# Small tiles merged, weights at another distance from the x tiles, and a copy ahead of a scan

## The chip, the cores and the metric

The kernel runs on one core of one Trainium2 chip. The metric is device time in microseconds, from the start of the program to its end; lower is better.

## What is computed

A linear attention with decay over r, k, v and w, followed by two feed-forward networks on its output:

```python
# attention: 4 x 8 heads, 768 tokens, 48 channels; state is 48 x 48 for each head
cur = u * k[t] outer v[t]
y[t] = r[t] @ (state + cur)
state = w[t] * state + k[t] outer v[t]
# first network, 3072 tokens x 384, inner width 2048
h = x @ w_in
x = where(h >= 1, h, where(h <= -1, 0, (h + 1)**2 / 4)) @ w_out
# second network, inner width 1536
g = x @ w_gate
out = (silu(g) * (x @ w_val)) @ w_out2
```

## The kernel before

The 3072 tokens are cut into 8 groups of 384, each of three windows of 128. The attention of a group is done by windows with matrix products: decays come from prefix and suffix scans along the tokens on VectorE, keys and receptances are scaled with them, and TensorE forms the products within a window and the state between windows. While TensorE works through the first network of group g, the attention of group g + 1 is slipped in between its tiles, and the scans of group g + 2 run on VectorE.

Precision: each weight and each activation is split into a high and a low part (names that end in hi and lo; fp32r), and a product is the sum of three matmuls, hi x hi, hi x lo and lo x hi. A matmul has a 128 x 128 weight as its stationary operand and streams 384 columns, the tokens of a group. So a tile of the first product (tokens into 128 inner channels, L1202) is 3 x 3 matmuls, and a tile of the second product (128 inner channels into the three accumulators, L1230) is 3 x 3 as well. The second network has two first products for each tile, gate and value.

The first network has 16 tiles (J1) in each group, the second 12 (J2). The order of work on each engine is written out by hand in slots: in slot (g, j) TensorE does the first product of tile j + 2, then attention work if any is due, then the second product of tile j. ScalarE and VectorE turn the hidden tile into ghi and glo in between. ScalarE writes ghi (L806), VectorE writes glo as the residual (L1055) and updates the gate (L1062). Synchronisation is by semaphores, which only count up; engines wait for a count.

At the end of a group the three accumulators are copied into `stage`, the first three slots of the tile `ring`: accumulators 0 and 2 by ScalarE (L828), accumulator 1 by VectorE (L1067, in `copy_out`). The second product of the next group's first tile takes the accumulators in the order 0, 2, 1 and waits for these copies, for accumulator 1 on the semaphore `ed`. SP then stores `stage` to memory (L610).

On VectorE the scans (L965, a reciprocal at L968, L975) have slots of their own. In group 0 they stand in slots 11, 14 and 15 (`SCAN_SLOTS_FIRST`), in later groups in 10, 13 and 14. So in group 0 a scan and the copy share slot 15.

Tiles of SBUF are placed by hand, one behind another: `place` takes the next free byte of a partition and rounds the size up to 32 bytes. The order is x (xhi, xlo, two of each, 4,608 bytes a tile), gate, ghi, glo (two of each, 1,536 bytes a tile), ring (10,752), constants (1,024), `w_checked` (1,024), three small tiles, then the weights of the first network (each family and part 24,576 bytes) and behind them the attention's tiles. When the attention is done, the second network's weights take the place of attention tiles and of first-network weights. The three small tiles belong to a guard on the decays: `beyond` holds sums that ScalarE writes for each window, VectorE adds them into `bad` (L1001), and one matmul with `ones` (L1345) sums over partitions for a flag.

Of the kernel before, what the change touches and what calls it, by code (L numbers as in the profile page):

```python
# [24 lines left out]
F32 = mybir.dt.float32  # L25
# [15 lines left out]
PR = 64 + D  # L41
KT = DM // P
J1, J2 = FF1 // P, FF2 // P
# [30 lines left out]
OPS_CHECK = 2 * NW  # L74
# [32 lines left out]
def first(g):  # L107
    return isinstance(g, int) and g == 0
# [10 lines left out]
def fills(g):  # L119
    return FIRST_FILLS if first(g) else FILLS  # L120
# [6 lines left out]
def build_program(nc, w_d, kr_d, tok_d, u_d, cst_d, w1i_d, w1o_d, w2g_d, w2v_d,  # L127
                  w2o_d, rs_d, ks_d, vs_d, ws_d, us_d, out_d, x2_d, ys_d):
    ctx = ExitStack()
    with ctx:  # L130
        at = [nc.sbuf_base + (-nc.sbuf_base) % 32]

        def place(name, shape, dt, offset=None):

            size = 2 if dt == mybir.dt.bfloat16 else 4
            for n in shape[1:]:
                size *= n
            if offset is None:
                offset = at[0]
                at[0] += (size + 31) // 32 * 32  # L140
            assert offset + size <= nc.sbuf_usable_end, (name, offset + size)
            return nc.alloc_sbuf_tensor_at(name, shape, dt, offset=offset), offset + size


        xhi = [place(f"xhi{i}", [P, KT, T], F32R)[0] for i in range(2)]
        xlo = [place(f"xlo{i}", [P, KT, T], F32R)[0] for i in range(2)]
        gate = [place(f"gate{i}", [P, T], F32)[0] for i in range(2)]
# [2 lines left out]
        ring, _ = place("ring", [P, KT + RING2, T], F32)  # L150
        stage = ring[:, 0:KT, :]
        cst, _ = place("cst", [P, 2 * P], F32)
# [1 line left out]


        checked, _ = place("w_checked", [PR, NPAIR * WIN], mybir.dt.bfloat16)
        beyond, _ = place("w_beyond", [PR, 2, OPS_CHECK + 2], F32)
        bad, _ = place("w_bad", [PR, OPS_CHECK + 1], F32)
        ones, _ = place("ones", [PR, 9], F32)
        ones = ones[:, 0:1]  # L160


        flag_at = (nc.sbuf_usable_end - 4) // 32 * 32
        flag, _ = place("flag", [1, 1], mybir.dt.int32, flag_at)
        w1_at = at[0]
        assert w1_at % 64 == 32
        w1i = [place(f"w1i{n}", [P, J1, KT * P], F32R)[0] for n in ("hi", "lo")]
        w1o_at = at[0]
        w1o = [place(f"w1o{n}", [P, J1, DM], F32R)[0] for n in ("hi", "lo")]
# [3 lines left out]
        w_at, _ = place("w_by_channel", [PR, NW, WROW + 1], F32)  # L173
        suf, _ = place("suf", [PR, NW, WROW], F32)
        kr, _ = place("k_r_by_channel", [PR, NW, 2, NPAIR, WIN], F32)
        last, _ = place("last_of_segment", [PR, WROW], F32)
        seed, _ = place("scan_seed", [PR, WROW], F32)
        tok, _ = place("r_k_v_by_token", [P, NW, 3, DM], F32)
        uu, _ = place("u_rows", [P, DM], F32)
# [3 lines left out]
        st, _ = place("state", [PR, NPAIR, D], F32)  # L183
        xn, _ = place("x_by_token", [P, NW, DM], F32)
        ring_b, _ = place("ring_b", [P, RING - KT - RING2, T], F32)
        dg, _ = place("diag", [P, NW, H], F32)
# [24 lines left out]
        for j in range(NA, J2):  # L211
            n = 2 + 6 * (j - NA)
# [50 lines left out]
        def state_pairs(w, parity):  # L263

            return 1 if parity == 1 and w == NW - 1 else NPAIR
# [22 lines left out]
        def bank_of(g, f):  # L288

            return (attb + hid + acc)[f % 8] if isinstance(g, int) and g == 0 else attb[f % NBANK]  # L290

        def twin(g, w):

            return (g * NW + w) % 2

        def y_two_ago(g, w):

            g2, w2 = divmod(g * NW + w - 2, NW)
            return g2 * NF + fill_no(g2, "Y", w2) + 1

        def cols(w):
            return slice(w * WIN, (w + 1) * WIN)
# [653 lines left out]
        def _(e):  # L956
# [61 lines left out]
            def drain(g, f, parity):  # L1018
                kind, w, n = fills(g)[f]
                src = bank_of(g, f)  # L1020
                if kind == "AT":
                    if n == 0:
                        decay_state(g, w, parity)
                    if first(g):
                        e.wait_ge(ld["cst"], 16)
                        e.wait_ge(zero_p, 9)
                    if g * NW + w >= 2:
                        e.wait_ge(fill, y_two_ago(g, w))
                    e.wait_ge(fill, g * NF + (f + 1))
                    mask = later.bitcast(U32).rearrange("p (a t) -> p a t", a=1).to_broadcast([P, 4, WIN])  # L1030
                    e.copy_predicated(att[twin(g, w)][n][:, :, :], mask, src[:, :].rearrange("p (a t) -> p a t", a=4))\  # L1031
                        .then_inc(at_out, 1)
                elif kind == "ST":
                    if first(g) and w == 0:
                        return
                    e.wait_ge(fill, g * NF + (f + 1))
                    e.wait_ge(st_dec, OPS_DECAY * (g * NW + w + 1))
                    n_pair = state_pairs(w, parity)
                    for i in range(2):
                        r0, c0 = 64 * i, D * i  # L1040
                        rows, pairs = slice(r0, r0 + D), slice(0, n_pair)
                        ps = src[rows, 0:n_pair * D].rearrange("p (a c) -> p a c", a=n_pair)
                        e.tensor_tensor(st[rows, pairs, :], ps, sbar[twin(g, w)][rows, pairs, c0:c0 + D], ALU.add).then_inc(st_out, 1)
                elif kind == "Y":
                    e.wait_ge(fill, g * NF + (f + 1))
                    e.wait_ge(diag_v, g * NW + w + 1)
                    e.tensor_tensor(xn[:, w, :], src[:, 0:DM], tok[:, w, 0, :], ALU.add).then_inc(y_out, 1)
                elif kind == "XT":
                    e.wait_ge(xh_out, g * NW + (w + 1))
                    e.tensor_tensor(xlo[parity][:, :, cols(w)], src[:, 0:DM].rearrange("p (k t) -> p k t", k=KT),  # L1050
                                    xhi[parity][:, :, cols(w)].bitcast(F32), ALU.subtract).then_inc(xl_out, 1)
# [12 lines left out]
            def copy_out(ph, g):  # L1064
                e.wait_ge(M["out", ph], (g + 2) * J[ph])
                e.wait_ge(M["st", ph], (g + 1) * 16)
                e.tensor_copy(stage[:, 1, :], acc[1][:, 0:T]).then_inc(M["ed", ph], 1)  # L1067
# [54 lines left out]
            def nxt(g, j, J_):  # L1122
                return (g, j) if j < J_ else (g + 1, j - J_)

            def slot(g, j, parity, next_half, after_next):
                last = isinstance(g, int) and g == NG - 1
                if not (last and j + 1 >= J1):
                    lo(1, *nxt(g, j + 1, J1))
                else:
                    lo(2, 0, 0)  # L1130
                if first(g) and j == XT_FIRST:
                    for f in win_slots(g)[j]:
                        drain(g + 1, f, 1 - parity)
                if not (last and j + 2 >= J1):
                    knee(*nxt(g, j + 2, J1))
                else:
                    swiglu(0, j + 2 - J1)
                if first(g):
                    if j in SCAN_FIRST:
                        scan_window(1, SCAN_FIRST[j])  # L1140
                    if j in SCALE_FIRST:
                        scale_window(1, SCALE_FIRST[j])
                    if j in DIAG_FIRST:
                        diag_sum(1, DIAG_FIRST[j])
                    if j == 6:
                        sum_w(1)
                elif next_half:
                    if j in SCALE_SLOTS:
                        scale_window(g + 1, SCALE_SLOTS[j])
                    if j in DIAG_SLOTS:  # L1150
                        diag_sum(g + 1, DIAG_SLOTS[j])
                if next_half and not (first(g) and j == XT_FIRST):
                    for f in win_slots(g).get(j, ()):
                        drain(g + 1, f, 1 - parity)
                if after_next:
                    if j in scan_slots(g):
                        scan_window(g + 2, scan_slots(g)[j])
                if after_next and j == SUM_SLOT:
                    sum_w(g + 2)
                if j == J1 - 1:  # L1160
                    copy_out(1, g)
                if last and j == 10:
                    split_x(0, 0)
                if last and j == 2:
                    e.wait_ge(w_sum, NG + 1)
                    e.tensor_reduce(bad[:, OPS_CHECK:OPS_CHECK + 1], bad[:, 0:OPS_CHECK], AX.X, ALU.add).then_inc(w_sum, 1)
                if last and j == 5:
                    e.wait_ge(w_tot, 1)
                    e.tensor_scalar(flag[:, :], attb[2][0:1, 0:1], 0.0, None, ALU.is_gt).then_inc(w_sum, 1)
# [253 lines left out]
```

## Time and profile before

| | |
|---|---|
| median of 3 runs | 992.36 us (992.11 to 992.6) |
| the profiled execution's own time | 992.52 us |
| its span, first to last instruction | 990.6 us |
| TensorE busy | 972.9 us, 98%, 6886 matmuls |
| VectorE busy | 519.5 us, 52% |
| ScalarE busy | 402.3 us, 41% |
| GpSimd busy | 163.5 us, 17% |
| data moved | 59.52 MB, mean 60 GB/s |

Busy time counts an instruction from its start to its end, and matmuls overlap each other, so TensorE's busy share tells that it always has something in flight and not how fast it goes. The pace is read from the distance of starts, or from the chain of work that ended last, in which each piece lasts until the next begins.

### The profile page before, as it was taken

The numbers are of one execution on the slowest core, as the hardware profiler recorded it, in microseconds if no ns is written. First come the engines' busy times: TensorE is split into PE (matmuls) and PEld (weight loads), VectorE is DVE, ScalarE is ACT, GpSimd is POOL, SyncE is SP. The second block draws the span as 40 slices with busy tenths as digits, with TensorE's granted clock in tenths as the row PEclk, the third lists the DMA queues.
The fourth block names the chain that finished last, engine by engine and source line by source line (L and its number), as shares of the span: only waits on it lengthen the run. The fifth ranks groups of instructions, "written<-read, shape, count | busy, mean of one in ns | idle before, by whom it ended". The sixth has DMA issues, their size and how long they took to land.

```text
span 990.6 us, 17480 instructions
## 1 busy us (share of the span) xinstructions
PE 972.9 (98%) x6886; PEld 954.7 (96%) x6886; DVE 519.5 (52%) x906; ACT 402.3 (41%) x841; POOL 163.5 (17%) x155
## 2 busy tenths in 40 slices
PE   6999999999999999999999999999999999999998
PEld 5899999999999999999999999999999999999997
DVE  8996666657576575764444433434333343334332
ACT  5665455454554554544665322222222222222222
POOL 6992210301102112020263200000000000000000
PEclk9999999999999999999999999999999999999999
DMA  9724212121222212100332100010100001010000
GB/s 303 238 66 132 85 55 86 53 86 52 87 77 62 87 43 95 68 2 1 132 108 88 57 17 32 1 49 1 48 0 29 19 0 48 0 48 0 24 1 25
DMA packets 23492, 59.52 MB, mean 60 GB/s; under 512 B 2688, under 2 KB 12032, under 8 KB 23424
## 3 DMA queue, kind: packets, MB, share of 16 engines
q1 hardware_dynamic: 23424, 58.59, 18.2%
q8 instruction: 46, 0.75, 0.3%
q14 instruction: 22, 0.18, 0.1%
HBM read 49.14 MB, written 9.44 MB: 59 GB/s over the span
## 4 chain that ended last, share of the span: by engine, by line
PE 94%; DVE 3%; issue 1%; ACT 1%; DMA 0%; DVEq 0%
PE bank L1202 50%; PE bank L1230 35%; PE bank L1258 2%; PE bank L1280 2%; PE bank L1275 1%; PE bank L1250 1%; DVE suf L965 1%; PE bank L1286 1%; PE bank L1267 1%; DVE att L1031 0%; DVE k_r_by_channel L990 0%; DVE k_r_by_channel L987 0%; DMA w_by_channel<-in_w_channel 0%; DVE glo L1055 0%; DVE gate L1062 0%
## 5 line engine op out<-in xcount | busy, mean ns | idle before, releaser
L806 ACT ACTIVATE ghi<-gate 128x384 fp32r<-128x384 f32 x224 | 117.3, 523 | 186.7 <-DVE gate L1074 95.6
L1055 DVE TENSOR_TENSOR glo<-gate,ghi 128x384 fp32r<-128x384 f32 x224 | 133.7, 597 | 113.2 <-ACT ghi L806 111.0
L1072 DVE TENSOR_TENSOR gate<-bank,gate 128x384 f32<-128x384 f32 x96 | 53.5, 557 | 223.2 <-ACT gate L925 223.2
L1202 PE MATMUL bank<-xhi,w2gv_alo 128*128 128x384 f32 x480 | 162.6, 339 | 0.0
L1202 PE MATMUL bank<-xlo,w2gv_ahi 128*128 128x384 f32 x480 | 162.5, 339 | 0.0
L1202 PE MATMUL bank<-xhi,w2gv_ahi 128*128 128x384 f32 x480 | 162.5, 339 | 0.0
L925 ACT ACTIVATE gate<-bank 128x384 f32<-128x384 f32 x96 | 47.3, 493 | 235.8 <-PE bank L1202 235.8
L1230 PE MATMUL bank<-ghi,w1ohi 128*128 128x384 f32 x384 | 134.8, 351 | 2.0 <-DVE ring L1067 1.1
L1202 PE MATMUL bank<-xhi,w1ihi 128*128 128x384 f32 x384 | 130.3, 339 | 1.3 <-issue 0.8
L1062 DVE SCALAR_TENSOR_TENSOR gate<-bank,gate 128x384 f32<-128x384 f32 x128 | 71.1, 555 | 112.4 <-ACT gate L815 112.4
L1230 PE MATMUL bank<-glo,w1ohi 128*128 128x384 f32 x384 | 130.0, 338 | 0.0
L1202 PE MATMUL bank<-xlo,w1ihi 128*128 128x384 f32 x384 | 129.9, 338 | 0.0
L1230 PE MATMUL bank<-ghi,w1olo 128*128 128x384 f32 x384 | 129.9, 338 | 0.0
L1202 PE MATMUL bank<-xhi,w1ilo 128*128 128x384 f32 x384 | 129.8, 338 | 0.0
L813 ACT ACTIVATE gate<-bank 128x384 f32<-128x384 f32 x128 | 62.8, 491 | 98.2 <-PE bank L1202 97.4
L1230 PE MATMUL bank<-ghi,w2ohi 128*128 128x384 f32 x288 | 97.5, 339 | 0.0
L1230 PE MATMUL bank<-ghi,w2olo 128*128 128x384 f32 x288 | 97.5, 339 | 0.0
L1230 PE MATMUL bank<-glo,w2ohi 128*128 128x384 f32 x288 | 97.5, 339 | 0.0
L1202 PEld LDWEIGHTS bank<-xhi,w2gv_ahi 128*128 128x128 f32 x480 | 90.0, 188 | 0.0
L1202 PEld LDWEIGHTS bank<-xlo,w2gv_ahi 128*128 128x128 f32 x480 | 90.0, 188 | 0.0
L1202 PEld LDWEIGHTS bank<-xhi,w2gv_alo 128*128 128x128 f32 x480 | 90.0, 188 | 0.0
L707 POOL TENSOR_TENSOR r_k_v_by_token<-r_k_v_by_token,diag 128x384 f32<-128x384 f32 x24 | 26.9, 1121 | 311.8 <-DVE diag L995 311.7
(95 smaller groups left out, 1580.4 us busy)
## 6 DMA issues: line engine op xcount, KB each, us to landing
r_k_v_by_token<-in_rkv_token SPq DMA_DIRECT2D x24, 576.0 KB, 5.0
k_r_by_channel<-in_kr_channel SPq DMA_DIRECT2D x24, 448.0 KB, 4.0
w_by_channel<-in_w_channel SPq DMA_DIRECT2D x24, 226.2 KB, 2.6
x_t<-ring SPq DMA_DIRECT2D x8, 576.0 KB, 2.8
x_raw<-x_t SPq DMA_DIRECT2D x8, 576.0 KB, 4.0
ring<-in_w_out SPq DMA_DIRECT2D x22, 192.0 KB, 2.5
out_t<-ring SPq DMA_DIRECT2D x7, 576.0 KB, 3.1
ring<-in_w_gate SPq DMA_DIRECT2D x12, 192.0 KB, 2.4
```

The costliest lines, as they stand in the source:

```text
L707: e.tensor_tensor(tok[:, w, 0, :].rearrange("p (h d) -> p h d", d=D), tok[:, w, 2, :].rearrange("p (h d) -> p h d", d=D), d_b, ALU.mult).t ...
L806: e.activation(ghi[j % 2][:, :], gate[j % 2][:, :], ACT.Copy).then_inc(M["hi", ph], 1)
L813: e.activation(q, hid[j % 2][:, 0:T], ACT.Relu, bias=0.5, scale=0.5).then_inc(M["q", 1], 1)
L925: e.activation(gate[j % 2][:, :], hid[j % 2][:, 0:T], ACT.Sigmoid).then_inc(M["q", 2], 1)
L965: e.tensor_tensor_scan(suf[:, w, ::-1], w_at[:, w, :0:-1], last[:, ::-1], 0.0, ALU.mult, ALU.max).then_inc(scan, 1)
L1055: e.tensor_tensor(glo[j % 2][:, :], gate[j % 2][:, :], ghi[j % 2][:, :].bitcast(F32), ALU.subtract)\
L1062: e.scalar_tensor_tensor(q, hid[j % 2][:, 0:T], 1.0, q, ALU.max, ALU.min).then_inc(M["g", 1], 1)
L1072: e.tensor_tensor(q, hid[j % 2][:, 0:T], q, ALU.mult).then_inc(M["t", 2], 1)
L1202: m = e.matmul(out, w_of(a, k), x_of(b_, k), start=start and i == 0, stop=stop and i == total - 1)
L1230: m = e.matmul(acc[k][:, 0:T], wo[a][:, j, k * P:(k + 1) * P], gs[b_][:, :], start=(j == 0 and i == 0), stop=(j == J[ph] - 1 and i == 2))
L1258: m = e.matmul(o[:, p * WIN:(p + 1) * WIN], kr[r, w, 0, p, :], kr[r, w, 1, p, :], start=True, stop=True)
L1280: m = e.matmul(out[t, h * D:(h + 1) * D], att[twin(g, w)][h % 2][:, h // 2, t], tok[:, w, 2, h * D:(h + 1) * D], start=(row_start and h == 0),
```

## The change

The three small tiles become one, `w_sums`, of 20 numbers, and `beyond`, `bad` and `ones` are parts of it. The weights are placed 96 bytes past the first x tile, counted by 256, with filler if needed; the test of the old place by 64 goes. On VectorE, in the last slot of group 0, the copy of accumulator 1 is issued ahead of the scan; in the other groups the order stays.

```diff
--- before.py
+++ after.py
@@ -142,6 +142,7 @@
             return nc.alloc_sbuf_tensor_at(name, shape, dt, offset=offset), offset + size
 
 
+        xhi_at = at[0]
         xhi = [place(f"xhi{i}", [P, KT, T], F32R)[0] for i in range(2)]
         xlo = [place(f"xlo{i}", [P, KT, T], F32R)[0] for i in range(2)]
         gate = [place(f"gate{i}", [P, T], F32)[0] for i in range(2)]
@@ -154,16 +155,18 @@
 
 
         checked, _ = place("w_checked", [PR, NPAIR * WIN], mybir.dt.bfloat16)
-        beyond, _ = place("w_beyond", [PR, 2, OPS_CHECK + 2], F32)
-        bad, _ = place("w_bad", [PR, OPS_CHECK + 1], F32)
-        ones, _ = place("ones", [PR, 9], F32)
-        ones = ones[:, 0:1]
+        sums, _ = place("w_sums", [PR, 3 * OPS_CHECK + 2], F32)
+        beyond = sums[:, 0:2 * OPS_CHECK].rearrange("q (b n) -> q b n", b=2)
+        bad, ones = sums[:, 2 * OPS_CHECK:3 * OPS_CHECK + 1], sums[:, 3 * OPS_CHECK + 1:3 * OPS_CHECK + 2]
+
+
+        W_STEP = 256
+        at[0] += (xhi_at + 96 - at[0]) % W_STEP
 
 
         flag_at = (nc.sbuf_usable_end - 4) // 32 * 32
         flag, _ = place("flag", [1, 1], mybir.dt.int32, flag_at)
         w1_at = at[0]
-        assert w1_at % 64 == 32
         w1i = [place(f"w1i{n}", [P, J1, KT * P], F32R)[0] for n in ("hi", "lo")]
         w1o_at = at[0]
         w1o = [place(f"w1o{n}", [P, J1, DM], F32R)[0] for n in ("hi", "lo")]
@@ -1152,12 +1155,14 @@
                 if next_half and not (first(g) and j == XT_FIRST):
                     for f in win_slots(g).get(j, ()):
                         drain(g + 1, f, 1 - parity)
+                if j == J1 - 1 and first(g):
+                    copy_out(1, g)
                 if after_next:
                     if j in scan_slots(g):
                         scan_window(g + 2, scan_slots(g)[j])
                 if after_next and j == SUM_SLOT:
                     sum_w(g + 2)
-                if j == J1 - 1:
+                if j == J1 - 1 and not first(g):
                     copy_out(1, g)
                 if last and j == 10:
                     split_x(0, 0)
```

## Rows read from the trace of the kernel before

**Rows 1.** The page: busy time of the engines, and TensorE's granted clock by slices.

```profile
PE 972.9 (98%) x6886; PEld 954.7 (96%) x6886; DVE 519.5 (52%) x906; ACT 402.3 (41%) x841; POOL 163.5 (17%) x155
...
PEclk9999999999999999999999999999999999999999
```

**Rows 2.** The page: the chain that ended last, by line.

```profile
PE bank L1202 50%; PE bank L1230 35%; PE bank L1258 2%; PE bank L1280 2%; PE bank L1275 1%; PE bank L1250 1%; DVE suf L965 1%; PE bank L1286 1%; PE bank L1267 1%; DVE att L1031 0%; DVE k_r_by_channel L990 0%; DVE k_r_by_channel L987 0%; DMA w_by_channel<-in_w_channel 0%; DVE glo L1055 0%; DVE gate L1062 0%
```

**Rows 3.** The chain in order of time (start, duration, what), second network.

```profile
529.62 3.18 PE bank L1202 x18
532.80 1.59 PE bank L1230 x9
...
978.00 3.18 PE bank L1202 x18
```

**Rows 4.** Groups by line: busy us, mean ns of one; one group of each three.

```profile
L1202 PE MATMUL bank<-xhi,w2gv_ahi 128*128 128x384 f32 x480 | 162.5, 339 | 0.0
...
L1230 PE MATMUL bank<-ghi,w1ohi 128*128 128x384 f32 x384 | 134.8, 351 | 2.0 <-DVE ring L1067 1.1 <-DVE glo L1055 0.9
L1202 PE MATMUL bank<-xhi,w1ihi 128*128 128x384 f32 x384 | 130.3, 339 | 1.3 <-issue 0.8 <-DVE gate L1062 0.5
...
L1230 PE MATMUL bank<-ghi,w2ohi 128*128 128x384 f32 x288 | 97.5, 339 | 0.0
...
L1202 PE MATMUL bank<-xhi,w2gv_bhi 128*128 128x384 f32 x96 | 32.5, 339 | 0.0
```

**Rows 5.** The chain in order of time, first network, group 1.

```profile
103.22 1.59 PE bank L1202 x9
104.81 1.59 PE bank L1230 x9
```

**Rows 6.** The waits: who waited for whom, us in total, times, longest.

```profile
PEld bank L1230 <- DVE ring L1067: 1.5, 1, 1.5
...
PE bank L1230 <- DVE ring L1067: 1.1, 1, 1.1
```

**Rows 7.** Groups by line: the instructions on the small tiles.

```profile
L1001 DVE TENSOR_TENSOR w_bad<-w_bad,w_beyond 112x6 f32<-112x6 f32 x8 | 2.3, 284 | 0.0
...
L1345 PE MATMUL bank<-ones,w_bad 112*1 112x1 f32 x2 | 0.2, 164 | 0.0
```

**Rows 8.** The chain in order of time: transposes of keys and of the attention's output.

```profile
111.17 0.39 PE bank L1250 x4
...
151.76 0.33 PE bank L1286 x3
```

**Rows 9.** The timeline of VectorE, end of group 0 (start, duration, engine, line, operation).

```profile
98.68 0.55 DVE L1062 SCALAR_TENSOR_TENSOR gate<-bank,gate 128x384 f32<-128x384 f32 x1
99.15 1.22 DVE L965 TENSOR_TENSOR_SCAN suf<-w_by_channel,last_of_segment 112x516 f32<-112x516 f32 x1
...
100.69 1.23 DVE L975 TENSOR_TENSOR_SCAN w_by_channel<-w_by_channel,scan_seed 112x516 f32<-112x516 f32 x1
101.84 0.53 DVE L1067 COPY ring<-bank 128x384 f32<-128x384 f32 x1
102.28 0.55 DVE L1055 TENSOR_TENSOR glo<-gate,ghi 128x384 fp32r<-128x384 f32 x1
```

**Rows 10.** The timeline of TensorE, end of group 0 and first tile of group 1.

```profile
98.30 0.34 PE L1230 MATMUL bank<-ghi,w1olo 128*128 128x384 f32 x1
...
100.77 0.34 PE L1230 MATMUL bank<-glo,w1ohi 128*128 128x384 f32 x1
100.95 0.33 PE L1230 MATMUL bank<-ghi,w1olo 128*128 128x384 f32 x1
102.42 0.44 PE L1230 MATMUL bank<-ghi,w1ohi 128*128 128x384 f32 x1 [1.14 <-DVE ring L1067]
102.70 0.34 PE L1230 MATMUL bank<-glo,w1ohi 128*128 128x384 f32 x1
```

**Rows 11.** The timeline of SP's DMA issues, end of group 0.

```profile
102.44 0.37 SPq L610 DMA_DIRECT2D x_t<-ring  x1
104.53 3.52 SPq L555 DMA_DIRECT2D w_by_channel<-in_w_channel  x2
```

## The prediction

> **What bounds the kernel.** I read the page's first two parts first. TensorE is busy 98% of the span, and its granted clock is 0.9 or more in every one of the 40 slices, so it runs at the upper of its two levels, 2.4 GHz, from end to end [rows 1]. The reader is to see that no other engine can be the bound: VectorE has 52%, ScalarE 41%. The chain that ended last says the same by line: L1202 (the first product of a tile) and L1230 (the second) hold 85% of the span, and the other lines of TensorE hold most of the rest [rows 2].
>
> Next I read the chain in order of time. In the second network it is nothing but pieces of 18 and 9 matmuls, 3.18 and 1.59 us long. From the piece at 529.62 to that at 978.00 lie 448.38 us, which is 94 slots of 4.77 us, each with 27 matmuls: 448.38 / (94 x 27) = 176.67 ns for a matmul of 384 columns [rows 3]. At one column per cycle of 2.4 GHz these columns last 160.0 ns, so each matmul carries 16.7 ns that its columns don't explain. How many there are comes from the groups by line, of which I show one of each three: 3 x (480 + 384 + 384 + 288 + 96) = 4896 [rows 4]. So one nanosecond on such a matmul is 4.9 us of the time, and the unexplained part is 4896 x 16.7 ns = 81.6 us. The first network's pieces of nine last the same 1.59 us [rows 5].
>
> Last I read the waits. TensorE waited once for VectorE's copy at L1067, for 1.1 us by its matmul and 1.5 us by its weight load [rows 6]; no later wait of TensorE is as long.
>
> **Part 1: where the tiles lie.** The three small tiles took 64 + 32 + 64 = 160 bytes of a partition; one tile of 20 numbers, 80 bytes, is rounded up to 96. What lies between the first x tile and these tiles (x, gate, ghi, glo, ring, constants, w_checked) is 40,448 bytes, which is 158 x 256. So the weights began 160 bytes by 256 past the x tiles; they now begin 96 past, and the filler that the new line adds is 0 bytes. Every weight tile, and x, ghi and glo as well, is a whole number of 256 bytes long, so all 4896 matmuls change from one distance to the other together. Tiles behind the weights move by the same 64 bytes; among themselves their distances stay.
>
> The instructions on the small tiles stay as many and as large: 8 additions of 284 ns and the matmul of one number at L1345, 164 ns [rows 7]. Their addresses and the step from one half of the sums to the other (8 numbers, now 6) change, and I cost that at nothing: VectorE, which does the additions, is idle 48% of the span. If that cover were gone they would cost at most their 2.3 us.
>
> The price of the new distance is not in the trace, since every large matmul in it has the old one. The bounds: the 16.7 ns vanish (81.6 us less), or as much again comes on top (81.6 us more). Nothing excludes either sign. The nearest rows are the transposes of the attention: they too load a stationary tile while another operand streams, and they have two other distances. By the sizes of the tiles k_r_by_channel lies 32 bytes by 256 past the identity that streams against it, and x_by_token 96. Four transposes of 112 columns lasted 0.39 us, three of 128 columns 0.33 us, so 0.87 and 0.86 ns a column at the two distances [rows 8]. They show no effect of the distance, and I take 0 ns. They are plain float32 at half the pace in columns, though, so they don't rule an effect out.
>
> The Trainium skill has two rules that pull apart here. "TensorE: Matmul & The Clock Gate", section "Step-by-step: what each phase is for", says that weights and the streaming operand are read through independent ports, so that a load doesn't slow the matmul that runs; by it the distance is worth nothing, the sum that I take. The same page's section "Wait — 56ns, not 53.3ns?" gives a warm matmul its columns at 2.4 GHz and about 2.5 ns; for 384 columns that would be 162.5 ns, which the measured 176.67 ns contradicts by 14.2 ns. By that second rule the 14.2 ns have a cause of their own, and a change that removed them would be worth 69.4 us, an estimate from that page's figure.
>
> **Part 2: the copy ahead of the scan.** In group 0, tile 15, VectorE did its scans (99.15 to 101.84), then the copy of accumulator 1 (101.84, 0.53 us) [rows 9]. TensorE needed the copy for the first tile of group 1: its matmul before the wait starts at 100.95, the next at 102.42, the one behind it at 102.70 [rows 10]. So the stall is 1.47 - 0.18 = 1.29 us, and 0.28 - 0.18 = 0.10 us more until weights load under matmuls again: 1.39 us. The copy's own condition, the last matmul of group 0, starts at 98.30 and lasts 0.34 us, so it is met at about 98.7. VectorE is then in the update of a gate that starts at 98.68 and lets the next instruction start at 99.15. The copy will start there without a wait and end by 99.7, against 101.13 when TensorE asks for it. The whole 1.39 us goes.
>
> What is late next? The scans come 0.5 us later, and the residual behind them (L1055, 102.28) starts when it started before, since the same work stands ahead of it [rows 9]. It ends at about 102.85. The matmuls that need it began at 104.81 [rows 5]; 1.39 us sooner they begin at 103.42, still 0.6 us behind it. Nobody asks for the scans' results before the next group. The copy issues no transfer, but the store of x that it releases on SP's queue left at 102.44 and can now leave near 99.7; the next issue there stands at 104.53, so nothing is queued behind it sooner [rows 11]. After that the chain is TensorE alone, so the gain lasts to the end.
>
> **The sum.** Profiled execution 992.52 us, its span 990.6, 1.9 us around it; the median is 992.36. 0 - 1.39 us from 992.36 gives 991.0 us. This is 0.14% less, below the 0.2% (2.0 us) that a measurement of this kernel can tell from no change.
>
> **The rivals.**
> - The new distance takes a part of the 16.7 ns away, 0.5 to 6 ns. For it: the part exists, nothing else in the trace names its cause, and the transposes at other distances have 3 to 4 ns over a cycle of 1.2 GHz per column (110 against 106.7, 97.5 against 93.3). Against it: matmuls on xhi, xlo, ghi and glo against five families of weights all have the same 176.7. 2 ns give 991.0 - 9.8 = 981.2 us; the ends are 988.6 and 961.6. From 0.13 ns on it counts as faster.
> - It takes most of it away, 6 to 16.7 ns: 961.6 to 909.4 us. Only the bound speaks for so much.
> - It adds to it, the other side: at L1202 and L1230 each matmul waits longer for an operand. 2 ns give 1000.8 us, the bound 1072.6. It decides from 0.69 ns on (1.39 + 2.0 us over 4896). No row shows a streaming matmul above 176.7, while rows show less per column, so this has less chance than the gain.
> - The copy's gain doesn't appear, since something else holds TensorE at the same place (the residual behind the scans, if they take longer in their new place): 992.4 us. Against it stand the 0.6 us.
>
> **How the numbers follow.** Forecast without an effect of the distance, 0.37; a part taken away 0.31; most taken away 0.14; added 0.13; gain of the copy lost 0.05. The predicted time is that of the first, 991.0 us, its own range 990.5 to 991.6. The range over the cases runs from 962 (all of the second case) to 1005 us (2.9 ns added); it leaves out the 0.14 and about 0.04 of the slower case. Faster by over 0.2%: 0.31 + 0.14, and 0.02 of the first case if the time falls by 0.6 us more than its sum, 0.47. Slower: 0.13. Within: 0.40.
>
> **What would show it.** The copy: L1067 at about 99.2, and TensorE's wait for it gone. The distance: pieces of 18 and 9 matmuls in the second network's chain of 3.18 and 1.59 us if it is worth nothing; each 0.01 us on a piece of nine is 1.1 ns on a matmul and 5.4 us on the time. The prediction is wrong if these pieces change, or if a new wait of TensorE stands between 99 and 107 us.

## The result, and the profile after

The changed kernel takes 976.13 us (median of 4 runs, 975.88 to 976.46) against 992.24 us before (4 runs): a ratio of 0.9838, 95% interval 0.9821 to 0.9855. So 16.1 us are gone, 1.6%. The time lies inside the stated range of 962 to 1005 us, but it is not that of the likeliest case: it is the first rival's, a part of the unexplained nanoseconds taken away.

The page of the changed kernel: busy time and the granted clock, then the costliest groups of TensorE that answer to [rows 4].

```profile
PE 958.0 (98%) x6886; PEld 940.0 (96%) x6886; DVE 517.8 (53%) x906; ACT 401.5 (41%) x841; POOL 163.4 (17%) x155
...
PEclk9999999999999999999999999999999999999999
...
L1207 PE MATMUL bank<-xhi,w2gv_ahi 128*128 128x384 f32 x480 | 161.3, 336 | 0.0
...
L1235 PE MATMUL bank<-ghi,w1ohi 128*128 128x384 f32 x384 | 133.8, 349 | 0.9 <-DVE glo L1058 0.9
...
L1235 PE MATMUL bank<-ghi,w2ohi 128*128 128x384 f32 x288 | 96.8, 336 | 0.0
```

The lines have moved down by up to five (L1202 is now L1207, L1230 is L1235, the copy L1067 is L1070). Counts, clock and TensorE's 98% are as in [rows 1], so this is no change of work or of clock. A matmul lasts 336 ns instead of 339, and the copy is no longer among what the second product waited for. Since matmuls overlap, the pace has to be read from the chain. The chain of the changed kernel in order of time, second network:

```profile
521.62 3.12 PE bank L1207 x18
524.74 1.56 PE bank L1235 x9
...
961.54 3.12 PE bank L1207 x18
```

These are the pieces of [rows 3], 3.12 and 1.56 us long where they were 3.18 and 1.59. From 521.62 to 961.54 lie 439.92 us, again 94 slots of 27 matmuls: 173.33 ns a matmul, 3.33 ns less than 176.67. Both are means. By the starts of single matmuls in the trace of the second network, the changed kernel's lie 173 or 174 ns apart throughout, while before they lay 174, 180, 175 and 178 ns apart, again and again in steps of four matmuls (within 1 ns). The operands repeat in steps of three (hi x hi, hi x lo, lo x hi), so the added time does not belong to one kind of product.

The first network's part is shorter than the count suggests. Two rows of the same chain:

```profile
45.38 1.80 PE bank L1235 x9
...
102.76 1.56 PE bank L1235 x9
```

The piece at 45.38 stood at 45.49 before: up to here the chain goes mostly through VectorE and ScalarE, and faster matmuls hardly help. The piece at 102.76 stood at 104.81 [rows 5], 2.05 us later; 1.4 us of this is the copy. The timeline of VectorE at the end of group 0:

```profile
98.21 0.55 DVE L1065 SCALAR_TENSOR_TENSOR gate<-bank,gate 128x384 f32<-128x384 f32 x1
98.67 0.55 DVE L1070 COPY ring<-bank 128x384 f32<-128x384 f32 x1
99.14 1.22 DVE L968 TENSOR_TENSOR_SCAN suf<-w_by_channel,last_of_segment 112x516 f32<-112x516 f32 x1
...
101.83 0.53 DVE L1058 TENSOR_TENSOR glo<-gate,ghi 128x384 fp32r<-128x384 f32 x1
```

The copy follows the gate at once, the scan follows the copy, and the residual at 101.83 is in good time for the second product that starts at 102.76.

### The profile page after: what moved, and what is told of

The parts are those of the page before. It is cut to its first block, busy times and chain, and to the rows that moved or that the text cites. A ratio compares the mean times of both kernels' runs of the same rounds, so it can differ in the third digit from the quotient of the medians.

```text
span 974.3 us, 17480 instructions
## 1 busy us (share of the span) xinstructions
PE 958.0 (98%) x6886; PEld 940.0 (96%) x6886; DVE 517.8 (53%) x906; ACT 401.5 (41%) x841; POOL 163.4 (17%) x155
## 4 chain that ended last, share of the span: by engine, by line
PE 96%; DVE 1%; DMA 1%; issue 1%; ACT 0%; SPq 0%; DVEq 0%; ACTq 0%
PE bank L1207 50%; PE bank L1235 36%; PE bank L1263 2%; PE bank L1285 2%; PE bank L1280 2%; PE bank L1255 1%; PE bank L1291 1%; PE bank L1272 1%; DMA w_by_channel<-in_w_channel 1%; DVE suf L968 0%; PE bank L1252 0%; DVE glo L1058 0%; DVE gate L1065 0%; DVE w_by_channel L978 0%; DVE k_r_by_channel L993 0%
## 5 line engine op out<-in xcount | busy, mean ns | idle before, releaser
L1207 PE MATMUL bank<-xhi,w2gv_ahi 128*128 128x384 f32 x480 | 161.3, 336 | 0.0
L1207 PE MATMUL bank<-xlo,w2gv_ahi 128*128 128x384 f32 x480 | 161.3, 336 | 0.0
L1207 PE MATMUL bank<-xhi,w2gv_alo 128*128 128x384 f32 x480 | 161.3, 336 | 0.0
L1235 PE MATMUL bank<-ghi,w1ohi 128*128 128x384 f32 x384 | 133.8, 349 | 0.9 <-DVE glo L1058 0.9
L1207 PE MATMUL bank<-xhi,w1ihi 128*128 128x384 f32 x384 | 129.2, 336 | 1.4 <-issue 0.8
L1235 PE MATMUL bank<-glo,w1ohi 128*128 128x384 f32 x384 | 129.1, 336 | 0.0
L1207 PE MATMUL bank<-xhi,w1ilo 128*128 128x384 f32 x384 | 129.1, 336 | 0.0
L1207 PE MATMUL bank<-xlo,w1ihi 128*128 128x384 f32 x384 | 129.0, 336 | 0.0
L1235 PE MATMUL bank<-ghi,w1olo 128*128 128x384 f32 x384 | 129.0, 336 | 0.0
L1235 PE MATMUL bank<-ghi,w2ohi 128*128 128x384 f32 x288 | 96.8, 336 | 0.0
L1235 PE MATMUL bank<-ghi,w2olo 128*128 128x384 f32 x288 | 96.8, 336 | 0.0
L1235 PE MATMUL bank<-glo,w2ohi 128*128 128x384 f32 x288 | 96.8, 336 | 0.0
L1207 PEld LDWEIGHTS bank<-xhi,w2gv_ahi 128*128 128x128 f32 x480 | 90.2, 188 | 0.0
L1207 PEld LDWEIGHTS bank<-xlo,w2gv_ahi 128*128 128x128 f32 x480 | 90.2, 188 | 0.0
L1207 PEld LDWEIGHTS bank<-xhi,w2gv_alo 128*128 128x128 f32 x480 | 90.2, 188 | 0.0
```

The lines of the kernel that those rows point to most:

```text
L1207: m = e.matmul(out, w_of(a, k), x_of(b_, k), start=start and i == 0, stop=stop and i == total - 1)
L1235: m = e.matmul(acc[k][:, 0:T], wo[a][:, j, k * P:(k + 1) * P], gs[b_][:, :], start=(j == 0 and i == 0), stop=(j == J[ph] - 1 and i == 2))
```

## Experiments

The theory: the distance, by 256 bytes, between the weights and the operand that streams against them sets the pace of every large matmul, and the copy adds 1.4 us. Rivals: the merged tile did it; the weights' own address did it; 96 is good because operands that lie far apart collide less. "Second network" below is the pace of its chain, worked out as above from the start of one slot to that of a later one.

**Each part alone.** The first kernel has the weights back at 160:

```diff
-        at[0] += (xhi_at + 96 - at[0]) % W_STEP
+        at[0] += (xhi_at + 160 - at[0]) % W_STEP
```

> The changed kernel with its weights put back to 160 bytes past the x tiles (by 256); the merged small tile and the moved copy stay. Theory A (the distance between weights and the streaming operand sets the pace of every large matmul): pieces of 9 matmuls return from 1.56 to 1.59 us, and only the copy's gain is left, 992.24 - 1.4 = 990.9 us. Theory B (something else of the edit, the merged tile or the smaller step between its halves, makes the matmuls faster): pieces stay at 1.56 us and the time near 976.1 us. If the copy's gain is eaten by a later wait, 992.2 us.

It took 991.35 us (11 runs) against 992.74 us (15 runs) of the kernel before on the same chip, a ratio of 0.9987 (0.9978 to 0.9996): 1.39 us. Its chain, in order of time, has the old pieces, but no stall among them:

```profile
98.60 1.59 PE bank L1207 x9
100.19 1.59 PE bank L1235 x9
101.78 1.59 PE bank L1207 x9
103.37 1.59 PE bank L1235 x9
```

and its timeline of VectorE shows the copy at 99.11, the first scan 0.42 us later than before, and the residual where it was [rows 9]:

```profile
99.11 0.55 DVE L1070 COPY ring<-bank 128x384 f32<-128x384 f32 x1
99.57 1.22 DVE L968 TENSOR_TENSOR_SCAN suf<-w_by_channel,last_of_segment 112x516 f32<-112x516 f32 x1
...
102.27 0.53 DVE L1058 TENSOR_TENSOR glo<-gate,ghi 128x384 fp32r<-128x384 f32 x1
```

So the merged tile, which this kernel keeps, is worth nothing that can be told: the time falls by what the stall was worth, and the pieces are the old ones. The second kernel has the new distance and the old order:

```diff
-                if j == J1 - 1 and first(g):
-                    copy_out(1, g)
                 if after_next:
                     if j in scan_slots(g):
...
-                if j == J1 - 1 and not first(g):
+                if j == J1 - 1:
                     copy_out(1, g)
```

> The changed kernel with VectorE's copy put back behind the scan; the new distance stays. Theory A: the pace stays at 1.56 us for 9 matmuls, TensorE waits again for the copy in group 0, and the time is 976.1 + 1.4 = 977.5 us. If the copy is worth nothing once the matmuls are faster, 976.1 us.

It took 977.38 us (5 runs), a ratio of 0.9847 (0.9834 to 0.9861), 15.4 us less than the kernel before. Its waits show the old stall again, a little longer, since TensorE now comes sooner:

```profile
PEld bank L1233 <- DVE ring L1070: 1.6, 1, 1.6
PE bank L1233 <- DVE ring L1070: 1.3, 1, 1.3
```

Its chain in order of time, behind that stall, shows something more:

```profile
104.06 1.59 PE bank L1233 x9
105.66 1.59 PE bank L1205 x9
...
125.22 1.56 PE bank L1233 x9
126.79 1.56 PE bank L1205 x9
```

The distance is 96 from end to end, and yet TensorE runs at the old pace for about 80 large matmuls, until 118 us; from 122 us on, behind more of the attention's work, it is back at 1.56 us. So the good distance does not exclude the slow pace, and the distance alone does not set it.

15.4 us and 1.4 us make 16.8, against 16.1 measured together; the runs of one kernel spread over 0.6 to 1.4 us, so the two add up as far as can be told.

**Distance or address.** Every tile lies 64 bytes further up, x included, so that the weights are at the old address by 256 and at the new distance:

```diff
+        at[0] += 64
         xhi_at = at[0]
```

> The changed kernel with every tile, x included, 64 bytes further up; the distance stays 96. The weights are then at the same address by 256 as in the kernel before. Theory A (the distance counts): 1.56 us for 9 matmuls, about 976 us. Rival (the weights' own address by 256 counts, not the distance): 1.59 us, about 991 us.

976.73 us in a single run, with the changed kernel's pieces in the chain. At this one shift the distance counts, and the weights' address alone does not.

```profile
564.22 3.12 PE bank L1208 x18
567.34 1.56 PE bank L1236 x9
```

**Other distances.** The same line as in the first experiment, with another number. The kernels below differ in it alone, apart from the one at 112.

> Distance 224 instead of 96, else as the changed kernel. If the distance counts by 128, it acts as 96 does: 1.56 us for 9 matmuls, 976 us. If it counts by 256, another pace; the kernel before had 160, so a pace between or beyond 1.56 and 1.59 us tells that the period is longer than 128. No theory here gives its size; one cycle of 1.2 GHz on each matmul is 4.1 us.

> Distance 0 by 256. Theory A as the runs so far have it: distance 96 gives 173.3 ns a matmul (208 cycles of 1.2 GHz), 160 gives 176.7 ns (212), 224 both of them in one run. Theory A1, loads and stream collide more often the nearer they lie: more than 212 cycles, 1000 us or above. Theory A2, only the half of 64 bytes counts beside a lock of the two streams: 212 cycles, 991 us.

> Distance 32 by 256, the last one that is 32 by 64. Theory A2 (a lock into one of two patterns): 173.3 or 176.7 ns, so 976 to 991 us, with no pace outside. Theory A1 (nearness): slower than distance 160, above 991 us.

> Distance 64 by 256. A1: between 32 and 96, so below 991 us. A2: the distances 0 and 64 by 64 behave as distance 0 does.

> Distance 192 by 256. So far 0, 32 and 96 give 173.33 ns a matmul in the second network, 64 gives 174.67, 160 and 224 give 176.67. Theory of a half (distances from 0 to 127 are good, from 128 on bad, with 64 in between by a mixed pattern): 176.67 ns, 985 to 991 us. Theory that only 160 and 224 are bad, the 32 by 64 class in the upper half: 173.33 ns, 976 us.

> Distance 128 by 256, the last of the eight steps of 32. So far 0, 32, 96 and 192 give 173.33 ns in the second network, 64 gives 174.67, 160 and 224 give 176.67. If slow distances go with the lower or the upper half by 256, 192 has already spoken against it. If every distance that is a multiple of 64 avoids 176.67 ns: 173.33 or 174.67 ns, 976 to 983 us. If 128 belongs with its neighbour 160: 176.67 ns, 986 to 991 us.

`place` gives addresses in steps of 32 bytes only. For 112, x, ghi and glo became slices of one tile, 16 bytes into it:

```diff
+        SH = 16 // 4
+        moving, _ = place("moving", [P, 4 * KT * T + 4 * T + 8], F32R)
+
+        def part(n, size):
+            return moving[:, SH + n:SH + n + size]
...
-        at[0] += (xhi_at + 96 - at[0]) % W_STEP
+        at[0] += (xhi_at + 16 + 112 - at[0]) % W_STEP
```

> x, ghi and glo start 16 bytes into one common tile, so that the weights are 112 past them, a distance between the steps of 32 tried so far. If only steps of 32 bytes matter: 173.33 ns and 976 us. If 16 bytes matter, another pace; a pace below 173.33 ns would make this kernel faster than both, each cycle of 1.2 GHz by 4.1 us, down to 160.0 ns (911 us) at the most.

| distance by 256 | us | second network, ns a matmul |
|---|---|---|
| 0 | 976.33 | 173.3 |
| 32 | 977.16 | 173.3 |
| 64 | 982.26 | 174.7 |
| 96 (the changed kernel) | 976.13 | 173.3 |
| 112 | 982.50 | 174.7 |
| 128 | 986.48 | 175.6 |
| 160 (copy alone) | 991.35 | 176.7 |
| 192 | 976.04 | 173.3 |
| 224 | 986.71 | 176.7 |

Apart from 96 and 160 these are single runs, on four chips on which the kernel before took 992.45 to 992.92 us. At 0 both expected times were missed, at 192 the second theory was met (173.33 ns, 976 us), and at 128 the pace lies between the two that were named. At 112 the pace is another one, but there the streaming operands also begin 16 bytes off a multiple of 32, so this row is not the distance alone. Nearness fails as an explanation: 0 and 32 are as good as 96, 64 between them is not. So do halves of 256 (192 is good), the class by 64 bytes (32 and 96 are good, 160 and 224 are not), and a period of 128 (96 and 224 differ). And 96 is nothing special: four of the eight steps of 32 have the same best pace in the second network, and none tried is below it. What the old place had was the slowest pace of all. How a pace is read, at 128 for example: its chain has the same piece of nine at 534.27 and at 932.43, 84 slots apart, and 398.16 / (84 x 27) = 175.6 ns.

```profile
534.27 1.58 PE bank L1235 x9
...
932.43 1.58 PE bank L1235 x9
```

The kernel at 224 shows more. Its second network has the slow pace, but its total is 4.6 us better than at 160. Rows of its chain in order of time, first network, two stretches:

```profile
149.51 0.33 PE bank L1291 x3
149.84 1.56 PE bank L1235 x9
151.40 1.56 PE bank L1207 x9
...
170.12 1.56 PE bank L1207 x9
171.68 0.39 PE bank L1255 x4
...
212.12 0.33 PE bank L1291 x3
212.45 1.59 PE bank L1235 x9
214.04 1.59 PE bank L1207 x9
...
233.12 1.59 PE bank L1207 x9
234.71 0.38 PE bank L1255 x4
```

The reader is to see both paces in one kernel, on the same lines and the same weights. Each stretch starts behind three transposes of the attention and runs unbroken for 22 us until the attention breaks in again; the first keeps 1.56 us for nine all the way, the second 1.59. So at this distance there are two patterns. They change from group to group: by the starts in the trace, the long stretches that begin near 150, 275 and 401 us have the fast one, those near 212, 338 and 463 us the slow one. Three transposes of the same kind stand ahead each time, so what chooses the pattern stays open. The kernel at 64 is mixed too, with stretches at 173.3, 174.7 and 176.7 ns, while at 160 every unbroken stretch of 35 matmuls or more was slow. The whole second network is one such stretch, so for 64 and 224 the table's pace is that of the pattern which this one run happened to keep.

**Which operands.** The low parts of the gate and value weights of ten of the twelve tiles lie 64 bytes further, at 160:

```diff
-            t, o = place(f"w2gv_a{n}", [P, NA, 2, KT * P], F32R, o)
+            t, o = place(f"w2gv_a{n}", [P, NA, 2, KT * P], F32R, o + (64 if n == "lo" else 0))
```

> Distance 96 for all but the low parts of ten of twelve gate and value tiles, which lie at 160. They are 480 of the 4896 stationary operands, and each is loaded while xlo streams. If the pace is set by the pair of operands that are read at once, these 480 times cost 4 cycles more, 1.6 us: 977.7 us, and the second product (L1235) stays at 1.56 us for 9. If a lock once lost stays lost, the second network falls to 1.59 us for 9 in its streaming part and the time goes to about 984.8 us (2592 matmuls by 3.33 ns). If only the weights' own matmul counts, 977.7 us too, but the longer gap is the one from the low part to the next high part.

975.69 us, and the chain still has pieces of 3.12 and 1.56 us:

```profile
563.35 3.12 PE bank L1207 x18
566.47 1.56 PE bank L1235 x9
```

All three expectations missed: one load in three of the second network's first product at the old distance costs nothing that this single run shows; the 1.6 us that were expected would have taken it to 977.7 us. In the last kernel ghi and glo are moved behind the attention's tiles, so that the first product has distance 96 and the second 160:

```diff
-        ghi = [place(f"ghi{i}", [P, T], F32R)[0] for i in range(2)]
-        glo = [place(f"glo{i}", [P, T], F32R)[0] for i in range(2)]
...
         dg, _ = place("diag", [P, NW, H], F32)
+        at[0] += (w1_at - 160 - at[0]) % W_STEP
+        ghi = [place(f"ghi{i}", [P, T], F32R)[0] for i in range(2)]
+        glo = [place(f"glo{i}", [P, T], F32R)[0] for i in range(2)]
```

> Distance 96 between weights and x, as in the changed kernel, but ghi and glo lie so that the weights are 160 past them: the first product (L1207) has the new distance, the second (L1235) the old one. If the pace is set by the pair of operands of the matmul at hand: L1235 at 1.59 us for 9, L1207 at 1.56; 1632 second-product matmuls by 3.33 ns make 976.1 + 5.4 = 981.5 us. If a streak must be long for the slow pattern to settle, the nine of L1235 stay near 1.56 and the time near 976 us. If the slow pattern, once there, stays, all go to 1.59 us and 991 us.

982.82 us. Its chain in order of time has the old pace in the second product and nearly the new one in the first:

```profile
562.98 3.13 PE bank L1208 x18
566.10 1.59 PE bank L1236 x9
567.69 3.13 PE bank L1208 x18
570.81 1.59 PE bank L1236 x9
```

So the slow pace came back in the runs of nine that have the old distance, although weights and x lie as in the changed kernel: the pair of weights and streaming operand counts, not the weights' place against other tiles. The time is 1.3 us over the 981.5 us worked out for this case, and no run says why.

## Why the prediction was right or wrong

- What bounds the kernel: right. From group 1 on (103 us) the chain holds TensorE alone, and a nanosecond on each large matmul was worth nearly what was worked out. Of 4.9 us a nanosecond, 3.33 ns would make 16.3 us; the layout alone gave 15.4. The second network gave its full 2592 x 3.33 ns = 8.6 us, the first 6.7 of 7.7 us, since its first tiles hang on VectorE and ScalarE and some 80 matmuls behind the stall kept the slow pace.
- The copy: right in each step. 1.39 us was the sum and 1.39 us the measurement of it alone, though the interval of that measurement runs from 0.4 to 2.2 us, so that the two agree to the digit is luck; the copy starts without a wait, the scan comes 0.42 us later (0.5 was said), the residual keeps its time, and the store leaves at 99.30 in the changed kernel (near 99.7 was said).
- The merged tile at nothing: right as far as can be told, as the kernel with the copy alone shows.
- The distance at nothing: this step failed. The likeliest case priced it at 0 ns, and it was worth 3.33 ns on a matmul of the second network and 15.4 us in all; by the prediction's own sign, the changed pieces, that case was wrong. The price came from the nearest rows, the transposes at distances 32 and 96 [rows 8], and these rows can't show it. The transposes move against the identity together with the weights: in the kernel at 224, x_by_token lies 160 past the identity, the distance at which the large matmuls are slow throughout, and three transposes still last 0.33 us (149.51 above). The prediction had left this open, since they run at half the pace in columns. The one thing the rows did show, 16.7 ns that the columns don't explain, spoke for the first rival, which had been given 0.31. The argument against that rival was empty: that all pairs of operands have the same 176.7 ns says nothing on the distance, as by the prediction's own count they all have the same one. The rival's range of 0.5 to 6 ns held the 3.33 ns; its worked time of 981.2 us took 2 ns. That the measured time lies inside the stated range comes from this rival, not from the sum.
- Most of the 16.7 ns taken away: wrong. At 173.33 ns there are still 13.3 ns over 160.0, and no distance tried changed that.
- The other side, an added cost: not seen; no distance of the nine is slower than 176.7 ns in the second network, so the old place left none of them worse.
- The two rules of the Trainium skill ("TensorE: Matmul & The Clock Gate"). By the section "Step-by-step: what each phase is for", a load of weights doesn't slow the matmul that runs; with the copy's effect taken out, moving the weights against the stream changed the large matmuls by 3.33 ns in the mean, so the operands' places do count, and here the measurement decides; that the load itself is what slows the stream is not shown. The section "Wait — 56ns, not 53.3ns?" has the columns and 2.5 ns, by an estimate from that figure 162.5 ns here; the best pace of these runs is 10.8 ns above it, and no run here, each with a load for every matmul, shows what the rest is.

What stays open is the mechanism. That two reads of one part of the memory collide would fit the dependence on the distance, but no run takes the load of weights away or looks at a single read, and the order of good and bad distances (0, 32, 96, 192 good) was not derived from anything. The trace has a load of 128 x 128 weights at 188 ns, before and after alike, longer than the pace of either kernel; so the loads may hold some of the 13.3 ns that are left, which no run tests. What chooses between the patterns at one distance is open as well. A period of 256 was not tested either: the kernels compared lie within one such step.

## What to carry to other kernels

Work out what a streaming matmul's columns last at the granted clock, and set the distance of starts beside it: what is left over, times the count, is the prize, and a range has to hold it even where no row has its price. Where operands are placed by hand, moving the stationary tiles against the streaming ones in the smallest steps that can be placed is a cheap scan, and the whole set should be tried, because good places don't lie next to each other: here half of the eight steps were equally good and the kernel stood on the slowest, one that was slow in every long stretch. A single run of a mixed distance can mislead, so the pace is to be read in more than one stretch. A row counts as evidence that an effect is absent only if it could have shown it.

## What the runs showed of the hardware that was not expected

The mean pace of matmuls of 384 fp32r columns at the full clock took the values 173.3, 174.7, 175.6 and 176.7 ns in the second network, by the distance between stationary and streaming operand, and steady to 0.01 us over pieces of nine. At distance 224 two of these paces appear in one run, and a long stretch of unbroken matmuls keeps the one it began with (1.56 or 1.59 us for nine over 22 us). Even at 96 a stretch behind a stall ran at 1.59 us. One load in three of the first product at a slow distance cost nothing (975.69 us), while nine matmuls in a row at it paid in full (1.59 us). Transposes of plain float32 kept their 0.33 us for three at the distance that is slow for the large matmuls.
